# The prologue of a fused attention and MLP kernel: loads in order of use, a plain fp32 low-rank path, and another order of the first products

## The chip, the cores and the metric

The kernel runs on one core of one Trainium2 chip. The metric is device time in microseconds (us) of one launch. A launch has five engines with queues of their own: TensorE (PE: matmuls and transposes through an identity matrix), VectorE (DVE), ScalarE (ACT), GpSimd (POOL) and SyncE (SP), which here issues DMAs only. ACT and POOL issue some DMAs too. Each engine works its queue strictly in order; waits on semaphores tie them together.

## The reference

```python
# attention without softmax, per batch b (8) and head h (8): seq 576, head_dim 64
kv  = einsum('bhsd,bhse->bhde', k, v)
out = einsum('bhsd,bhde->bhse', q, kv)
x   = out / sqrt(mean(out*out, -1) + 1e-6) * g_norm          # then laid out as (8, 576, 512)
# block 1: low rank over the sequence (U 576x32, V 32x576), then an MLP 512 -> 2048 -> 512
u = x + (x.transpose(0,2,1) @ U @ V).transpose(0,2,1)
x = u + maximum(u @ w_ch1, 0) @ w_ch2
# block 2: h = gelu(x @ w_in), 1024 wide, halves u and v; v layer-normed, mixed over the
# sequence by w_sg (576x576) + b_sg; result x + (u * v) @ w_out
```

All inputs and the output are fp32.

## The kernel before, in words

The work is staged. The attention is cut into 32 units; unit m is one pair of heads of one batch (four units to a batch). For each unit PE multiplies k by v (`k_v`, L1439), transposes q (`q_transposed`, L1423), multiplies q by kv (`attention`, L1450 and L1452). ACT copies the result out of PSUM, squares it (L736) and takes a root (L740); DVE sums (L1011) and scales (L1018) to the normalised tile y. Then comes the low-rank part: PE forms a = U^T y (`low_rank`, L1458), DVE splits a into a high and a low part (`a_split`), and PE transposes y and adds V^T a (`u_transposed`, L1423 and L1469); ACT moves that to SBUF with g_norm (`u_evacuated`, L756), and SP stores it to DRAM (`store_u`, L388).

The MLP matmuls are run as three products of high and low parts in the type fp32r (L1418, L1419, L1420: hi by hi, hi by lo, lo by hi), and blocked in seven combined products in place of eight. So activations and weights need sums and differences first (`x_sum`, `w1_sums`), a rounded high part from ACT (`x_high` L771, `w1_high` L761) and a low part from DVE (`x_low` L1073, `w1_low` L1046). The up projection of batch t is a tile of 56 steps; a step is six matmuls; 14 steps are a group of the weight w_ch1 (four groups, 0 to 3). Between the steps of tile t the units of batch t+1 are worked at fixed places: after step 0 of the first tile the attention of unit 4 and k by v of unit 5; in every group low rank after step 7, `u_transposed` after step 10, the next unit's attention and k by v after step 13.

Before the first tile lies the prologue: units 0 to 3, the preparation of weight group 0, and k by v of unit 4. Its order is written out by hand in one loop `for m in range(HP)` on each engine. The raw k, v and q of units 0 to 4 come over SP's queue (q of unit 0 over ACT's), U, V and w_ch1 over POOL's. POOL issues w_ch1 in three parts: part 0 is group 0, part 1 is group 1, part 2 is groups 2 and 3; each part is eight DMAs, released by a count of finished k by v products. The sums of weight groups 0 and 1 are made by DVE, those of groups 2 and 3 by POOL. In SP's queue the loads of unit 5 (k and v, then q in 32-column blocks, L376) stand between the store of unit 0 and the stores of units 1 to 3. The first low part of an activation (`x_low(0, 0, 0)`) waits for the stores of units 0 and 1, because it overwrites what they read.

After the up projection come the down projection and block 2; they are not touched.

## Time and profile before

| what | value |
|---|---|
| median of three timed runs | 1295.93 us (1294.95 to 1296.66) |
| the profiled execution: its own time, and its span | 1293.79 us, 1292.0 us |
| PE busy | 1261.8 us, 98% of the span |
| DVE, ACT, POOL busy | 824.7 us, 543.8 us, 101.3 us |
| first matmul of the kernel, first up-projection product | 7.34 us, 45.93 us |
| attention of unit 5 (after step 13 of the first tile) | 67.14 us |
| read from and written to device memory | 109.47 MB, 66.06 MB |

The span is the time between the first and the last instruction in the trace; the execution's own time is what the timer gives around it. A share of busy time is a mean over all stages. The stage at issue here is the first 5% of the span.

### The profile page before, as it was taken

What the parts mean: (1) busy time and instruction counts of PE and PEld (TensorE: products, weight loads), DVE (VectorE), ACT (ScalarE), POOL (GpSimd) and SP (SyncE); (2) the same over time, 40 slices, a digit from 0 to 9 for tenths busy, and PEclk for the clock granted to TensorE, in tenths of its full rate; (3) what the DMA queues carried; (4) which work ended last, traced back from release to release, by engine and by line L of the source; (5) the groups of instructions that cost most, each with busy time, mean ns of one, the idle gap of its engine ahead of it and who ended that gap; (6) DMA issues with size and microseconds to landing.
All of it is one profiled execution on the core that took longest, in us unless ns stands there. A gap on an engine that the chain in (4) does not pass through costs nothing.

```text
span 1292.0 us, 21466 instructions
## 1 busy us (share of the span) xinstructions
PE 1261.8 (98%) x8311; PEld 1221.4 (95%) x8311; DVE 824.7 (64%) x1196; ACT 543.8 (42%) x867; POOL 101.3 (8%) x107
## 2 busy tenths in 40 slices
PE   5799999999999999999999999999999999999998
PEld 5699999999999999999999999998898998998987
DVE  4886465645555558998888889976634535336343
ACT  4565454445455445654535444534322212223121
POOL 7210000000000000000000000002302012022000
PEclk9899999999999999999999999999999999999999
DMA  9555665655565456671735446362342241340321
GB/s 236 131 154 154 176 164 157 156 147 156 173 166 157 129 189 242 215 260 62 265 101 191 170 154 225 100 196 57 96 85 66 62 113 50 72 111 31 57 58 41
DMA packets 285365, 178.61 MB, mean 138 GB/s; under 512 B 197456, under 2 KB 255840, under 8 KB 285296
## 3 DMA queue, kind: packets, MB, share of 16 engines
q1 hardware_dynamic: 282336, 172.82, 46.3%
q0 software_dynamic: 1600, 4.56, 1.3%
q8 instruction: 45, 0.74, 0.2%
q10 hardware_dynamic: 1360, 0.30, 0.1%
q14 instruction: 24, 0.20, 0.0%
HBM read 109.47 MB, written 66.06 MB: 136 GB/s over the span
## 4 chain that ended last, share of the span: by engine, by line
PE 93%; DVE 3%; issue 1%; ACT 1%; SPq 1%; DMA 0%; POOL 0%; DVEq 0%; ACTq 0%; POOLq 0%
PE ps L1418 28%; PE ps L1420 28%; PE ps L1419 27%; PE ps L1439 3%; PE ps L1450 2%; PE ps L1423 2%; PE ps L1458 1%; PE ps L1681 1%; PE ps L1684 1%; PE ps L1469 1%; PE ps L1452 1%; DVE w_lo L1180 0%; SPq L376 0%; DVE y L1018 0%; DVE x_lo L1073 0%
## 5 line engine op out<-in xcount | busy, mean ns | idle before, releaser
L1418 PE MATMUL ps<-x_hi,w 128*128 128x288 f32 x896 | 268.0, 299 | 3.5 <-DVE x_lo L1073 2.7
L1419 PE MATMUL ps<-x_lo,w 128*128 128x288 f32 x896 | 264.6, 295 | 0.0
L1420 PE MATMUL ps<-x_hi,w 128*128 128x288 f32 x896 | 264.3, 295 | 0.0
L1418 PE MATMUL ps<-r_hi,w_hi 128*128 128x384 f32 x672 | 224.6, 334 | 0.1
L1420 PE MATMUL ps<-r_hi,w_lo 128*128 128x384 f32 x672 | 224.5, 334 | 0.0
L1419 PE MATMUL ps<-r_lo,w_hi 128*128 128x384 f32 x672 | 224.5, 334 | 0.0
L880 ACT ACTIVATE r_hi<-hb 128x768 fp32r<-128x768 f32 x168 | 142.4, 848 | 168.5 <-PE ps L1420 164.7
L1418 PEld LDWEIGHTS ps<-x_hi,w 128*128 128x128 f32 x896 | 168.5, 188 | 5.6 <-issue 4.3
L1420 PEld LDWEIGHTS ps<-x_hi,w 128*128 128x128 f32 x896 | 168.8, 188 | 0.0
L1419 PEld LDWEIGHTS ps<-x_lo,w 128*128 128x128 f32 x896 | 168.7, 188 | 0.0
L1208 DVE TENSOR_TENSOR r_lo<-hb,r_hi 128x768 fp32r<-128x768 f32 x120 | 114.5, 955 | 30.0 <-ACT r_hi L880 30.0
L1418 PEld LDWEIGHTS ps<-r_hi,w_hi 128*128 128x128 f32 x672 | 126.2, 188 | 0.4 <-DVE r_lo L1206 0.4
L1420 PEld LDWEIGHTS ps<-r_hi,w_lo 128*128 128x128 f32 x672 | 126.2, 188 | 0.0
L1419 PEld LDWEIGHTS ps<-r_lo,w_hi 128*128 128x128 f32 x672 | 126.2, 188 | 0.0
L780 ACT ACTIVATE h_st<-ps 128x576 f32<-128x576 f32 x128 | 81.4, 647 | 55.7 <-PE ps L1420 51.2
L1084 DVE TENSOR_TENSOR h_st<-ps,h_st 128x576 f32<-128x576 f32 x96 | 71.9, 750 | 46.9 <-PE ps L1420 46.6
L1355 DVE SCALAR_TENSOR_TENSOR vs<-ps,glcol,bias_bc 128x576 f32<-128x576 f32 x32 | 26.1, 816 | 86.3 <-PE ps L1684 86.3
L1418 PE MATMUL ps<-ws_hi,vn_hi 128*128 128x288 f32 x256 | 75.6, 295 | 0.0
L1418 PE MATMUL ps<-x_hi,wu_hi 128*128 128x288 f32 x256 | 75.6, 295 | 0.0
L1420 PE MATMUL ps<-x_hi,wu_lo 128*128 128x288 f32 x256 | 75.5, 295 | 0.0
L1420 PE MATMUL ps<-ws_hi,vn_lo 128*128 128x288 f32 x256 | 75.4, 295 | 0.0
L1419 PE MATMUL ps<-ws_lo,vn_hi 128*128 128x288 f32 x256 | 75.4, 294 | 0.0
(156 smaller groups left out, 2347.1 us busy)
## 6 DMA issues: line engine op xcount, KB each, us to landing
hT_scratch<-h_st SPq DMA_DIRECT2D x64, 576.0 KB, 4.6
hb<-hT_scratch SPq DMA_DIRECT2D x24, 1536.0 KB, 7.5
uT_scratch<-x_raw SPq DMA_DIRECT2D x32, 288.0 KB, 2.3
x_st<-uT_scratch SPq DMA_DIRECT2D x24, 384.0 KB, 3.5
x2T_scratch<-x_st SPq DMA_DIRECT2D x24, 384.0 KB, 7.0
x_raw<-x2T_scratch SPq DMA_DIRECT2D x8, 1152.0 KB, 5.6
xt_in<-x2T_scratch SPq DMA_DIRECT2D x144, 64.0 KB, 2.5
k_raw<-in_k SPq DMA_DIRECT2D x64, 128.0 KB, 4.0
```

Of the source, the lines that this page charges most:

```text
L780: nc.scalar.activation(h_st[:, g % 2, :, {0: 0, 1: 3, 2: 1, 6: 2}[idx], :], ps[:, o:o + 2, 0:SH], ACT.Copy).then_inc(s_cp, 1)
L880: nc.scalar.activation(r_hi[:, n % RING], piece(h_source(i), q_), ACT.Relu if i in (3, 6) else ACT.Copy).then_inc(s_hhi, 1)
L1084: nc.vector.tensor_tensor(c, ps[:, o:o + 2, 0:SH], c, ALU.add).then_inc(s_ad, 1)
L1208: ins = nc.vector.tensor_tensor(lo, x, hi, ALU.subtract)
L1355: nc.vector.scalar_tensor_tensor(vs[:, c % 2, :].rearrange("p (a m) -> p a m", a=2), us_tile(c), glcol[:, c:c + 1], bias_bc[:].rearrange(" ...
L1418: mm(dst, ws[0], xs[0], start=first, stop=False, skip_group_check=chained)
L1419: mm(dst, ws[0], xs[1], start=False, stop=False, skip_group_check=chained)
L1420: return mm(dst, ws[1], xs[0], start=False, stop=last, skip_group_check=chained)
L1423: return mm(dst, src, identF[:], is_transpose=True, start=start, stop=stop)
L1439: ins = mm(ps[:, bx, at_:at_ + P], k_raw[n][:, j], v_raw[n][:, :, j, :], start=(j == 0), stop=(j == NJ - 1))
L1450: ins = mm(ps[:, bx, j * P:(j + 1) * P], qT[:, j], kv[:], start=True, stop=True)
L1452: mm(ps[:, by, 0:P], qT[:, JM], kv[:], start=True, stop=True).then_inc(s_out, 1)
```

## The change

Only the prologue and the first tile change. Seven things:

1. PE runs 12 transposes of the identity before it has data (`WARM`), and in each unit the transpose of q now comes before k by v. ACT takes a root of a constant right after its first two DMA issues, and q of units 0 and 1 are issued by ACT, q of unit 2 by POOL.
2. SP loads k and v of units 0, 1 and 2 first; unit 3 waits for the k by v of unit 1 (two finished).
3. POOL issues, after the first k by v: q of unit 2, V, then part 0 of w_ch1. Part 1 waits for four finished k by v as against three, part 2 for six as against four.
4. The low rank of units 0 to 3 runs in plain fp32 (`low_rank_first`, `a_split_first`): five matmuls of 128x128 on y itself by U repeated three times (`U_rep`). The high and low parts of y, the copy of a's second half and its addition are gone for these four units.
5. Attention of unit 4 comes before the first product, k by v of unit 5 behind step 5, and its evacuation is spread over the first steps (`first_steps`).
6. On DVE the first activation sums are interleaved with the normalisation of unit 4; `w1_low` of group 0 comes in the same loop.
7. SP stores units 0 and 1 before it loads k and v of unit 5, then units 2 and 3, then q of unit 5. POOL's sums of group 2 also wait for DVE's sums of group 1.

```diff
-            load_next(HP + 1)
-            for r in range(1, HP):
-                store_u(0, r)
+            store_u(0, 1)
+            load_kv((HP + 1) // HP, (HP + 1) % HP, HP + 1, 0)
+            store_u(0, 2)
+            store_u(0, 3)
+            load_q_blocks(HP + 1)
...
+            pool.wait_ge(s_kv, 1)
+            for h in range(2):
+                pool.dma_start(q_raw[2][:, 0:JM, h, :], ...).then_inc(s_q[2], 16)
...
             pool.wait_ge(s_kv, 1)
             load_w1(0, slice(0, 2))
-            pool.wait_ge(s_kv, 3)
+            pool.wait_ge(s_kv, HP)
             load_w1(1, slice(2, 4))
-            pool.wait_ge(s_kv, HP)
+            pool.wait_ge(s_kv, HP + 2)
             load_w1(2, slice(4, NPAIR))
+            pool.wait_ge(s_wsum[1], 4)
...
+            def a_split_first(m):
+                a = ps[:, 3, 0:P]
+                dve.wait_ge(s_a, m + 1)
+                nc.vector.tensor_copy(a_aug[:], a).then_inc(s_ahi, 1)
+                dve.wait_ge(s_ahi, m + 1)
+                o = slice(R, 2 * R)
+                nc.vector.tensor_tensor(a_aug[o, :], a[o, :], a_aug[o, :].bitcast(F32), ALU.subtract).then_inc(s_alo, 1)
...
+            def low_rank_first(m):
+                pe.wait_ge(s_y, m + 1)
+                for j in range(NJ):
+                    ins = mm(ps[:, 3, 0:P], U_rep[:, j], y_first[m % 3][:, j], start=(j == 0), stop=(j == NJ - 1))
+                ins.then_inc(s_a, 1)
...
+            for n in range(WARM):
+                ins = transpose(ps[:, 4, 0:P], identF[:], True, True)
             q_k_v_first(0)
...
-                if first and k == 0:
-                    attention_and_next(m)
+                if first and k == 5:
+                    pe.wait_ge(s_o, 2 * (HP + 1))
+                    k_v(HP + 1, BY, 1, 2, P)
```

On SP the place is the end of the prologue's queue, from q of unit 4 on. `uT_scratch` rows are the stores of units, `k_raw` and `v_raw` the loads of unit 5, `q_blk` its q. Before:

```order
L366 DMA q_raw<-in_q 64x2x64
L388 DMA uT_scratch<-x_raw_79 128x2x288 [waits uT_evacuated]
L351 DMA k_raw<-in_k 128x4x64 [waits kv_done]
L351 DMA k_raw<-in_k 128x4x64
L354 DMA k_raw<-in_k 64x2x64
L356 DMA v_raw<-in_v 128x2x256
L358 DMA v_raw<-in_v 64x2x64
L376 DMA q_blk<-in_q 32x18x32 [waits qT_done]
L376 DMA q_blk<-in_q 32x18x32 x3
L388 DMA uT_scratch<-x_raw_79 128x2x288 [waits uT_evacuated] x3
```

And after:

```order
L369 DMA q_raw<-in_q 64x2x64
L391 DMA uT_scratch<-x_raw_79 128x2x288 [waits uT_evacuated] x2
L354 DMA k_raw<-in_k 128x4x64 [waits kv_done]
L354 DMA k_raw<-in_k 128x4x64
L357 DMA k_raw<-in_k 64x2x64
L359 DMA v_raw<-in_v 128x2x256
L361 DMA v_raw<-in_v 64x2x64
L391 DMA uT_scratch<-x_raw_79 128x2x288 [waits uT_evacuated] x2
L379 DMA q_blk<-in_q 32x18x32 [waits qT_done]
L379 DMA q_blk<-in_q 32x18x32 x3
```

The second store now stands ahead of nine loads, and q of unit 5 behind all four stores.

On POOL the place is from the identity matrix on; `w_raw_59` is the raw weight of group 0, `w_raw_60` that of groups 1 to 3. Before:

```order
L646 DMA U_raw<-in_moe_U 128x4x32
L647 DMA U_raw<-in_moe_U 64x32
L649 DMA V_raw<-in_moe_V 32x576 x4
L656 DMA w_raw_59<-in_moe_w_ch 128x2x128 [waits kv_done]
L656 DMA w_raw_59<-in_moe_w_ch 128x2x128 x7
L656 DMA w_raw_60<-in_moe_w_ch 128x2x128 [waits kv_done]
```

And after:

```order
L651 DMA U_raw<-in_moe_U 128x4x32
L652 DMA U_raw<-in_moe_U 64x32
L659 DMA q_raw_90<-in_q 128x4x64 [waits kv_done]
L659 DMA q_raw_90<-in_q 128x4x64
L660 DMA q_raw_90<-in_q 64x2x64
L662 DMA V_raw<-in_moe_V 32x576 x4
L669 DMA w_raw_59<-in_moe_w_ch 128x2x128 [waits kv_done]
L669 DMA w_raw_59<-in_moe_w_ch 128x2x128 x7
```

Seven issues (three of q, four of V) now stand between the first k by v and the first weight DMA, where there was none.

On DVE the place is the end of the prologue, from the sum over the squares of unit 3 on. Before:

```order
L1022 TENSOR_TENSOR y_hl<-y,y_hl 128x5x128 [waits y_hi_ready]
L1053 TENSOR_TENSOR x_raw_79<-x_raw_79 128x576 [waits uT_evacuated]
L1026 TENSOR_TENSOR part<-ps,part 128x128 [waits a_part]
L1028 CAST a_aug<-part 128x128 [waits a_sum]
L1031 TENSOR_TENSOR a_aug<-part,a_aug 32x128 [waits a_hi_ready]
L1046 TENSOR_TENSOR w_0_55<-w_raw_59,w_0_55 128x1792 [waits w1_hi_ready]
L1073 TENSOR_TENSOR x_lo_77<-x_raw_79,x_hi 128x576 [waits uT_stored1,uT_stored0,x_hi_ready]
L1057 TENSOR_TENSOR x_raw_79<-x_raw_79 128x576 [waits u_sums_ready,uT_evacuated]
```

And after:

```order
L1048 TENSOR_TENSOR y_92<-y_92,rstd 128x640 [waits rstd_ready]
L1089 TENSOR_TENSOR w_0_55<-w_raw_59,w_0_55 128x1792 [waits w1_hi_ready]
L1096 TENSOR_TENSOR x_raw_79<-x_raw_79 128x576 [waits uT_evacuated]
L1066 CAST a_aug<-ps 128x128 [waits a_done]
L1069 TENSOR_TENSOR a_aug<-ps,a_aug 32x128 [waits a_hi_ready]
L1116 TENSOR_TENSOR x_lo_77<-x_raw_79,x_hi 128x576 [waits uT_stored1,uT_stored0,x_hi_ready]
L1100 TENSOR_TENSOR x_raw_79<-x_raw_79 128x576 [waits u_sums_ready,uT_evacuated]
L1116 TENSOR_TENSOR x_lo_77<-x_raw_79,x_hi 128x576 [waits x_hi_ready]
L1041 TENSOR_REDUCE ssum<-sq 128x10 [waits squares_ready]
```

The low part of y (L1022) is gone, the split of a has two instructions in place of three, the second weight low part has moved ahead of the last split, and the sum for unit 4 has moved in among the activation sums.

## Rows read from the trace of the kernel before

**Rows 1.** Waits of PE, whole span: what it waited for, us, times, longest.

```profile
PE ps L1439 <- DMA v_raw<-in_v: 7.3, 1, 7.3
PE ps L1450 <- ACT qT L710: 5.8, 4, 2.1
...
PE ps L1418 <- DVE x_lo L1073: 2.7, 1, 2.7
PE ps L1458 <- DVE y_hl L1022: 2.3, 1, 2.3
```

**Rows 2.** Windows: length, busy PE, PEld, DVE, ACT, POOL, PEclk, DMA share, GB/s.

```profile
14.00:15.00 1.00, 1.00 (x7) 1.00 (x7) 0.00 (x0) 0.85 (x3) 1.00 (x2) 0.54 0.97 266
...
67.00:100.00 33.00, 32.88 (x260) 32.67 (x259) 25.76 (x31) 21.76 (x36) 5.86 (x4) 1.00 0.56 158
```

**Rows 3.** Timeline of PE: start, us, engine, line, operation, tiles, [idle before].

```profile
7.34 2.47 PE L1439 MATMUL ps<-v_raw,k_raw 128*128 128x128 f32 x10 [7.34 <-DMA v_raw<-in_v]
...
45.93 0.58 PE L1418 MATMUL ps<-x_hi,w 128*128 128x288 f32 x1 [2.73 <-DVE x_lo L1073]
...
67.14 1.05 PE L1450 MATMUL ps<-kv,qT 128*128 128x128 f32 x8
...
69.77 0.29 PE L1418 MATMUL ps<-x_hi,w 128*128 128x288 f32 x1
...
75.37 0.29 PE L1418 MATMUL ps<-x_hi,w 128*128 128x288 f32 x1
```

**Rows 4.** Timeline of POOL: its DMA issues, and its first weight sum.

```profile
3.64 0.92 POOL L646 DMA_DIRECT2D U_raw<-in_moe_U  x1
4.55 0.55 POOL L647 DMA_DIRECT2D U_raw<-in_moe_U  x1
5.10 1.98 POOL L649 DMA_DIRECT2D V_raw<-in_moe_V  x4
10.11 5.67 POOL L656 DMA_DIRECT2D w_raw<-in_moe_w_ch  x8 [3.03 <-PE ps L1439]
...
26.90 5.95 POOL L656 DMA_DIRECT2D w_raw<-in_moe_w_ch  x8 [0.16 <-issue]
54.34 1.29 POOL L286 TENSOR_TENSOR w_raw<-w_raw 128x512 f32<-128x512 f32 x1 [21.50 <-PE ps L1420]
```

**Rows 5.** Tile w_raw, 0 to 60 us: time from issue to landing.

```profile
DMA to landing us min/median/max: 3.7/5.3/8.1
```

**Rows 6.** Groups of DVE, 0 to 46 us: busy us, mean ns, idle before.

```profile
L1046 DVE TENSOR_TENSOR w<-w_raw,w 128x1792 fp32r<-128x1792 f32 x2 | 4.1, 2026 | 0.6 <-ACT w L761 0.5
L1018 DVE TENSOR_TENSOR y<-y,rstd 128x640 f32<-128x640 f32 x4 | 3.3, 825 | 0.1
L1011 DVE TENSOR_REDUCE ssum<-sq_first 128x10 f32<-128x640 f32 x4 | 3.3, 815 | 3.8 <-ACT sq_first L736 3.8
L1031 DVE TENSOR_TENSOR a_aug<-part,a_aug 32x128 fp32r<-32x128 f32 x4 | 1.1, 281 | 0.1
L1073 DVE TENSOR_TENSOR x_lo<-x_raw,x_hi 128x576 fp32r<-128x576 f32 x1 | 0.8, 757 | 1.7 <-DMA uT_scratch<-x_raw 1.7
L286 DVE TENSOR_TENSOR w_raw<-w_raw 128x512 f32<-128x512 f32 x1 | 0.7, 686 | 0.0
```

**Rows 7.** Groups of ACT, 0 to 46 us.

```profile
L761 ACT ACTIVATE w<-w_raw 128x1792 fp32r<-128x1792 f32 x2 | 3.4, 1684 | 0.0
L756 ACT ACTIVATE x_raw<-ps,gcol 128x576 f32<-128x576 f32 x4 | 2.9, 727 | 2.3 <-PE ps L1469 2.3
L706 ACT ACT_TABLE_LOAD x1 | 1.3, 1283 | 10.8 <-PE ps L1423 10.8
L740 ACT ACTIVATE stdv<-ssum,eps_col 128x10 f32<-128x10 f32 x4 | 1.2, 303 | 3.9 <-DVE ssum L1011 3.9
```

**Rows 8.** Timeline of SP's queue: the issue of unit 5's q.

```profile
38.12 4.12 SPq L376 DMA_DIRECT2D q_blk<-in_q  x4
```

**Rows 9.** Timeline of DVE: the scaling of unit 4, with POOL at work.

```profile
54.52 1.79 DVE L1018 TENSOR_TENSOR y<-y,rstd 128x640 f32<-128x640 f32 x1
```

More of the change, by code:

```diff
@@ L54 @@
 NO = NJ
+WARM = 12
 NXT = 3
@@ L152, in build @@
     q_raw = [q_raw] + [at(f"q_raw{i}", [P, NJ, 2, HD], F32) for i in range(1, HP)]
[L153 removed]
+    y_first = [at(f"y{i}", [P, NJ, P], F32) for i in range(1, 3)] + [y]
     sq_first = at("sq_first", [P, NJ, P], F32)
[L155 to L156 removed]
+    U_rep = at("U_rep", [P, NJ, 4 * R], F32)
     assert cursor[0] <= phase_end
+    V_raw = at("V_raw", [P, S], F32, offset=x_hi_off + 2 * SH * 4)
+    U_raw = at("U_raw", [P, NJ, R], F32, offset=x_hi_off + 3 * 2 * SH * 4)
     wsize = FH * DH * 4
@@ L787, in x2_high, with load_q @@
                 nc.scalar.activation(x2_hi[par][:, :, 0:n], x2_raw[:, :, 0:n], ACT.Copy).then_inc(s_x2hi, 1)
-            for h in range(2):
-                act.dma_start(q_raw[0][:, 0:JM, h, :], q[0, h, 0:SM, :].rearrange("(j p) d -> p j d", p=P)).then_inc(s_q[0], 16)
-            act.wait_ge(s_zero, 1 + 3 * HP)
-            act.dma_start(q_raw[0][0:ST, JM, :, :], q[0, 0:2, SM:S, :].rearrange("h p d -> p h d")).then_inc(s_q[0], 16)
+            def load_q(m):
+                for h in range(2):
+                    act.dma_start(q_raw[m][:, 0:JM, h, :], q[0, 2 * m + h, 0:SM, :].rearrange("(j p) d -> p j d", p=P)).then_inc(s_q[m], 16)
+                if m == 0:
+                    act.wait_ge(s_zero, 1)
+                    nc.scalar.activation(stdv[:, 0:1], eps_col[:], ACT.Sqrt).then_inc(s_pass, 1)
+                    act.wait_ge(s_zero, 2 + 3 * HP)
+                act.dma_start(q_raw[m][0:ST, JM, :, :], q[0, 2 * m:2 * m + 2, SM:S, :].rearrange("h p d -> p h d")).then_inc(s_q[m], 16)
+            for m in range(2):
+                load_q(m)
             for n in range(2):
                 act.dma_start(gcol[HD * n:HD * (n + 1), :], g_norm.rearrange("(p o) -> p o", o=1)).then_inc(s_g, 16)
-            act.wait_ge(s_zero, 3 * HP + 6)
             q_copy(0, 0, first=True)
@@ L817, in _, with first_steps @@
             u_evacuated(2, 2, 4, 0, -1)
-            a_part(3, 3)
             x_high(0, 0, 1)
+            attn_copy(HP, BX, BY)
             u_evacuated(3, 3, 4, 0, -1)
-            for idx in range(2, NI):
-                x_high(0, 0, idx)
+            squares(HP, sq)
             X_HIGH_AT = (26, 34, 53)
             X_HIGH_THEN = (1, 2, 3, 6)
+            def first_steps():
+                x_high(0, 0, 2)
+                copied(0, 1)
+                std(HP)
+                x_high(0, 0, 3)
+                copied(0, 3)
+                x_high(0, 0, 4)
+                y_high(HP)
+                x_high(0, 0, 5)
+                copied(0, 5)
+                kv_copy(HP + 1, BY, P)
+                x_high(0, 0, 6)
             def up_tile(t, par, first=False, end=False):
-                for k in range(STEPS):
+                if first:
+                    first_steps()
+                for k in range(6 if first else 0, STEPS):
                     g, idx, s_ = step(k)
@@ L1103, in _ @@
                 kv_copy(m + 1, 2)
+                if m == HP - 1:
+                    a_split_first(m - 1)
                 normalise(m, ym)
-                if m:
-                    a_split(m - 1, 3)
-                y_low(m, ym)
+                if m == 0:
+                    low_rank_factors()
+                elif m < HP - 1:
+                    a_split_first(m - 1)
                 if m == 1:
                     w1_sums(dve, nc.vector, 0)
-                if m == 2:
-                    w1_low(0)
+                elif m > 1:
+                    w1_low(m - 2)
             x_sum(0, 0, 1)
-            a_split(3, 3)
-            w1_low(1)
+            a_split_first(3)
             x_low(0, 0, 0)
-            for idx, low_ in ((2, 1), (6, 2), (4, 3)):
-                x_sum(0, 0, idx)
-                x_low(0, 0, low_)
+            x_sum(0, 0, 2)
+            x_low(0, 0, 1)
+            sums(HP, sq)
+            x_sum(0, 0, 6)
+            x_low(0, 0, 2)
+            normalise(HP)
+            x_sum(0, 0, 4)
+            y_low(HP)
+            x_low(0, 0, 3)
+            x_low(0, 0, 4)
             w1_sums(dve, nc.vector, 1)
@@ L1123, in up_tile @@
             def up_tile(t, par, first=False, end=False):
-                for k in range(STEPS):
+                for k in range(5 if first else 0, STEPS):
                     g, idx, s_ = step(k)
@@ L1139, in up_tile @@
                         a_split(m, BX)
-                    if k in X_LOW_THEN[2 if first else 0:]:
+                    if k in X_LOW_THEN[3 if first else 0:]:
                         x_low(t, par, 2 + X_LOW_THEN.index(k))
@@ L1485, in _ @@
                 if m > 1:
+                    if m == 2:
+                        pe.wait_ge(s_low, 2)
+                    else:
+                        pe.wait_ge(s_uev, m - 2)
                     u_transposed(m - 2, 4, y_first[m - 2])
@@ L1509, in attention_step @@
                 m = HP * (t + 1) + r
-                if first and k == 0:
-                    attention_and_next(m)
+                if first and k == 5:
+                    pe.wait_ge(s_o, 2 * (HP + 1))
+                    k_v(HP + 1, BY, 1, 2, P)
                 if at_ == LOW:
```

75 lines of the change are left out of this document (40 added, 35 removed).

## The prediction, made before the changed kernel had run

> **What bounds the kernel now.** I read the waits of PE first, then the windows, then the timelines and groups of each engine over the first 70 us. The waits of PE [rows 1] show the only sizeable idle time of the launch: 7.3 us until the first k and v have landed, 5.8 us for the copy of transposed q, 2.7 us in one piece ahead of the first up-projection product, 2.3 us for the low rank of unit 4. From 67 us on PE is full: 32.88 of 33.00 us, at granted clock 1.00 [rows 2]. So what is saved before the attention of unit 5, at 67.14 us [rows 3], goes through to the end of the launch one for one, and nothing else can be saved. I therefore forecast one moment, the start of that attention, and carry its shift to the end.
>
> **How the early part hangs together.** The first product starts at 45.93 us [rows 3]. The reader is to see in its row that PE came free 2.73 us earlier and was released by a low part x_lo on DVE, and in DVE's group of that operation that DVE itself had waited 1.7 us for the store of the activation [rows 6]. That store was late because in SP's queue it stood behind the nine loads of unit 5, the four of q alone taking 4.12 us to issue from 38.12 us on [rows 8]. Further back it is a chain over DVE and ACT: the sums of weight group 0, then by turns the reduction of a unit's squares, its root, its evacuation and a weight high part on ACT, and a weight low part on DVE. PE mostly waits for that.
>
> **The change, part 1: when weight group 0 lands.** Before, POOL was released by the first k by v at 10.11 us and issued the eight DMAs in 5.67 us [rows 4], 0.71 us each, so the last began at 15.1; with the median of 5.3 us to landing [rows 5] it had landed at 20.4. DVE waited for nothing before its first sum [rows 6].
>
> After, the first k by v ends a little earlier. It took 2.47 us at the low clock level from 7.34 us on [rows 3]. Now the transpose of q and at best a PE at the high level come first; k's tail no longer waits for all 13 fills. I bound the release by 9.1 us (matmuls at the high level, half of 2.47) and 10.9 us (low level, transposes 0.8 us before them) and take 9.8. Then POOL issues q of unit 2, whose three DMAs I price like those of U, 0.92 + 0.92 + 0.55, and V, 1.98 [rows 4]: 4.4 us together, to 14.2 us. The last of the eight weight DMAs begins 4.96 us later, at 19.2, and lands 3.7 to 8.1, median 5.3 us after that [rows 5]: 22.9 to 27.3, taken as **24.5 us**. DVE will have finished the split of unit 0's a by about 21.5 us and will then stand at this wait, with every later DVE instruction queued behind it: the reduction, copy of kv and scaling of unit 2, and through them PE's attention of unit 3. This is the new wait that the change adds, and the first place where I expect its gain to be given back in part.
>
> At this place a rule of the Trainium skill speaks against the change. The row first: eight POOL issues took 5.67 us and another eight 5.95 us with DVE busy nearly throughout [rows 4]. "SBUF — State Buffer", section "SBUF: two separate sides", says that a DMA from GpSimd's queue has its descriptors written by the GpSimd cores, and that a DVE copy from SBUF to SBUF can lock them out for as long as it runs. By that rule the moved q and V could be held by each of the three new copies of U; by the rows one issue is lengthened by 5% at most.
>
> **Part 2: from the weight to the first product.** On the path from 24.5 us stand, with durations from [rows 6, 7]: the four sums of group 0, 4 x 0.686 less their overlap, 2.5; the reduction of unit 2, 0.8; ACT's root, evacuation of unit 0 and weight high part, 0.30 + 0.73 + 1.68 = 2.7; DVE's weight low part, 2.0; reduction of unit 3, 0.8; again root, evacuation, high part, 2.7; low part, 2.0; the sum for activation 1, 0.75; the split of unit 3's a, two instructions at 0.28, 0.55; PE's five transposes and two matmuls for unit 3, 1.0. Together 15.9 us, so the first product at **40.4 us**, 5.5 us earlier. What went out beside that path: per unit a high part and a copy on ACT, a low part (128x640, as the 0.825 of L1018) and an addition on DVE, four units, 3.3 + 1.2 us of DVE time of which some 4 us lay on the old path. The stores of units 0 and 1 are issued by about 34.5 us, so the 1.7 us wait goes; next late is the split of unit 3's a, by which DVE stands before its first x_lo. The fp32 low rank costs PE about what k by v costs, which is beside the DVE path and priced at nothing; if that cover went, four times 0.3 us. The attention of unit 4 runs in PE's wait, at nothing too.
>
> **Part 3: from the first product to the attention of unit 5.** Before: 67.14 - 45.93 = 21.2 us. PE's own work there is 14 steps, and a step takes (75.37 - 69.77) / 7 = 0.80 us at full clock [rows 3], 11.2 us; with k by v, low rank and the transposes of unit 4 about 14.1 after the change. DVE needs more: evacuation of unit 3 on ACT, 0.7; eight activation sums and low parts at 0.7 to 0.757, 5.8; reduction, reciprocal and scaling of unit 4, 1.9; ACT's two high parts that stand between, 1.3; y's low part 0.8; the sums of group 1, 2.6; the transpose of q, one h addition, 1.4; split of a, 0.8; then on PE the transposes of unit 4 and three steps, 3.4. That is 18.7 by the row durations; I take 18.5, since neighbours overlap by some 0.07 us each. So **58.9 us**, 8.2 us earlier than 67.14. PE idles about 4 us in this stretch, in pieces of one to two us.
>
> The clock: in the window 14 to 15 us the granted clock is 0.54 of 2.4 GHz [rows 2], that is mostly the 1.2 GHz level, after PE had stood idle about 2 us before its first attention; the first product after 2.73 us of idle took 0.58 in place of 0.29 us [rows 3]. The new gaps are shorter, so a fall costs at most one or two of them, and most of it lies under DVE's path: between 0 and 1.7 us, taken as nothing beyond the rounding above.
>
> **Part 4: what comes back.** POOL's sums of group 2 began at 54.34 us [rows 4], and DVE's scaling of unit 4 at 54.52 took 1.79 us [rows 9] in place of 0.825 [rows 6]. They went on together, and PE's 2.3 us wait for unit 4's low part [rows 1] came of it. After the change part 2 is issued only from the k by v of unit 5 on, about 47 us, in 5.95 us, and lands near 58. The sums then run beside DVE's last weight low part of group 1 and the scaling of unit 5, which PE needs at steps 15 and 21. Each DVE instruction with two SBUF inputs may lose up to 1 us there, from two to four of them; PE's slack is about 1 us. Between 0 and 4 us, taken as **1.0**.
>
> **Sum.** 8.2 - 1.0 = 7.2 us. The profiled execution took 1293.79 us around a span of 1292.0; it would take 1286.6. The median of the timed runs is 2.1 us above the profiled one, so on that scale 1295.93 - 7.2 = **1288.7 us**.
>
> **Rivals.** (A) POOL's queue is later than I take it: release at 10.9, landing after 8.1 us, some issues held up. Weight group 0 is then there at 29 us and the gain shrinks by 4.5 to 2.7 us, 1293.2 us. For it: landings of up to 8.1 us, with the DMA engines at a share of 0.97 in the window 14 to 15 us [rows 2]. Against it: the same queue now carries fewer bytes in the same time. (B) It lands before DVE comes for it at 21.5 us, and no sum on POOL costs PE anything: 3.0 + 1.0 more, a gain of 11.2, 1284.7 us. For it: POOL's DMAs compete with less, since unit 3 and half of w_ch1 wait. Against it: it needs a landing faster than the quickest seen, or a q of unit 2 that issues faster than U. (C) Slower than before: weight groups 2 and 3, now released by the sixth k by v in place of the fourth, come too late for step 28. Part 2's last DMA begins near 52.5 us; at worst it lands at 60.7; four sums on POOL take 5.2 us alone [rows 4] and about twice that in collision with DVE, so they end between 63 and 71. Then 1.68 and 2.03 us [rows 6, 7] must fit in before step 28 at about 74 us. The point from which it decides is sums ending after 70; to turn the result over, at 1298.6 us (2.7 above), they would have to end at 80. Against it: nothing in the rows reaches that far. (D) The 12 transposes do not do what their name says. No stretch of this trace has transposes alone. PE would then stay at 1.2 GHz through the first k by v, the release is 10.4 to 10.9 us, and the gain is 6.4 us, 1289.5 us: inside my case. The Trainium skill, "TensorE: Matmul & The Clock Gate", "Part 4: PE-mode transpose", says that such transposes do not count as a busy PE; by that rule the granted clock stays low until after the first matmuls on real data.
>
> **Numbers.** My case, with D in it: 68%, 1286.4 to 1290.9 us. A: 16%. B: 10%. C or another late piece: 6%. A measurement here can tell 0.2%, 2.6 us, from no change. Faster: 68 + 12 of A + 10 = 90%; within 0.2%: 4 of A + 1 of C = 5%; slower: 5%. The range leaves out the far end of B and C: 1284.8 to 1292.8 us.
>
> **What would show it.** In the profile after: POOL's first w_raw issue at about 14 us; DVE idle before its first w_raw sum, ended by the DMA, for up to 3 us; the first product near 40.4 us, released by PE's own queue or by the split of a; no wait of x_lo for uT_scratch; the attention that follows step 13 near 59 us; PE full from there except near steps 15 and 21. It is wrong if PE waits for w1's low part at step 28, if the first product comes after 44 us, or if the shift at 67 us is not the shift at the end.

## The result, and the profile after

The changed kernel ran in 1287.68 us (median of 4 runs, 1286.45 to 1289.27) against 1295.44 us (4 runs, 1294.64 to 1296.66) for the kernel before on the same chip: a ratio of 0.994, interval 0.9923 to 0.9957, or 7.8 us less. The forecast was 1288.7 us, the range 1284.8 to 1292.8.

Waits of PE after, whole span (what it waited for, us, times, longest), against [rows 1]:

```profile
PE ps L1502 <- issue: 4.3, 2, 2.4
PE ps L1475 <- POOL identF L649: 3.4, 1, 3.4
PE ps L1470 <- DVE x_lo L1116: 2.4, 3, 1.6
```

The waits for the copy of transposed q and for the high and low parts of y have left the top of the list. Apart from the 3.4 us until POOL has made the identity matrix, the largest single one is now 2.4 us, before an attention. Timeline of PE after, the lines that answer to [rows 3]:

```profile
7.66 2.12 PE L1491 MATMUL ps<-v_raw,k_raw 128*128 128x128 f32 x10
...
28.80 1.13 PE L1502 MATMUL ps<-kv,qT 128*128 128x128 f32 x8 [2.42 <-issue]
...
33.23 1.32 PE L1491 MATMUL ps<-v_raw,k_raw 128*128 128x128 f32 x10
...
41.66 0.32 PE L1470 MATMUL ps<-x_hi,w 128*128 128x288 f32 x1
...
60.15 1.05 PE L1502 MATMUL ps<-kv,qT 128*128 128x128 f32 x8
```

The first product is at 41.66 us, 4.27 earlier than before, the attention of unit 5 at 60.15, 6.99 earlier. POOL after, answering to [rows 4]:

```profile
10.07 1.53 POOL L659 DMA_DIRECT2D q_raw<-in_q  x2 [4.54 <-PE ps L1491]
11.60 0.61 POOL L660 DMA_DIRECT2D q_raw<-in_q  x1
12.20 2.01 POOL L662 DMA_DIRECT2D V_raw<-in_moe_V  x4
14.20 5.68 POOL L669 DMA_DIRECT2D w_raw<-in_moe_w_ch  x8
...
49.44 5.96 POOL L669 DMA_DIRECT2D w_raw<-in_moe_w_ch  x8 [18.23 <-PE ps L1491]
...
63.00 1.30 POOL L289 TENSOR_TENSOR w_raw<-w_raw 128x512 f32<-128x512 f32 x1 [7.60 <-DMA w_raw<-in_moe_w_ch]
```

Weight group 0 is issued from 14.20 us on, and POOL's sums of group 2 begin at 63.00 in place of 54.34. On DVE [rows 6, 9] one sees the new wait, and that the work on unit 4 is stretched no more:

```profile
24.84 0.69 DVE L289 TENSOR_TENSOR w_raw<-w_raw 128x512 f32<-128x512 f32 x1 [2.52 <-DMA w_raw<-in_moe_w_ch]
...
34.59 0.47 DVE L1138 COPY kv<-ps 64x64 f32<-64x64 f32 x2 [1.06 <-PE ps L1491]
...
35.70 0.29 DVE L1066 CAST a_aug<-ps 128x128 fp32r<-128x128 f32 x1 [0.64 <-PE ps L1527]
...
40.70 0.76 DVE L1116 TENSOR_TENSOR x_lo<-x_raw,x_hi 128x576 fp32r<-128x576 f32 x1
...
46.28 0.82 DVE L1048 TENSOR_TENSOR y<-y,rstd 128x640 f32<-128x640 f32 x1
```

The scaling of unit 4 takes 0.82 us (before 1.79), and x_lo waits for no store. The split of unit 5's a, at 70.59 us, is still stretched (1.28 us in place of 0.28), with POOL's sums beside it. Windows after (length, busy PE, PEld, DVE, ACT, POOL, PEclk, DMA share, GB/s), against [rows 2]:

```profile
30.00:31.00 1.00, 0.69 (x5) 0.44 (x3) 0.63 (x3) 1.00 (x2) 1.00 (x2) 0.50 0.84 269
60.00:93.00 33.00, 32.90 (x261) 32.70 (x260) 26.60 (x31) 21.73 (x36) 12.90 (x8) 1.00 0.66 173
```

From 60 us on PE is full again, with POOL at work for 12.90 of 33 us. At 30 us its granted clock is 0.50, the 1.2 GHz level, right after the wait of 2.42 us.

**From 60 us to the end.** The profiled execution of after took 1288.74 us around a span of 1286.9. That is 5.1 less span than before's 1292.0, though the attention of unit 5 had moved by 7.0. The shift was still 6.7 us at a wait of PE in block 2 for the low part ws_lo, of the same length in both (2.14 and 2.15 us): it ends at 888.73 us before and at 882.00 after. One window behind it, in before and then in after:

```profile
890.00:892.00 2.00, 2.00 (x18) 2.00 (x17) 1.42 (x2) 0.83 (x2) 0.00 (x0) 1.00 0.01 2
```

```profile
884.00:886.00 2.00, 2.00 (x10) 2.00 (x10) 0.97 (x2) 0.18 (x1) 0.00 (x0) 0.50 0.03 8
```

The code there is the same. In this execution of after the clock was at its lower level and 10 matmuls passed in 2 us in place of 18; the shift fell to 5.2 us. Of the fourteen traces of this study eight show the fall at that place and six do not. Kernels built on the changed one and kernels built on the one before are among both, so I take it to belong to an execution and not to the change; no kernel was traced both with the fall and without it. From the end of that wait to the end of the span take 404.8 to 404.9 us with the fall and 403.3 to 403.4 without, so by itself it makes single executions differ by some 1.5 us. So below, early moments are read in the traces and totals only in medians.

### The profile page after: what moved, and what is told of

It reads as the page before. It is cut to its first block, busy times and chain, and to the rows that moved or that the text cites. A ratio compares the mean times of both kernels' runs of the same rounds, so it can differ in the third digit from the quotient of the medians.

```text
span 1286.9 us, 21517 instructions
## 1 busy us (share of the span) xinstructions
PE 1263.7 (98%) x8343; PEld 1222.5 (95%) x8343; DVE 817.9 (64%) x1189; ACT 539.3 (42%) x859; POOL 104.2 (8%) x111
## 4 chain that ended last, share of the span: by engine, by line
PE 94%; DVE 3%; DMA 1%; issue 1%; POOL 1%; ACT 1%; ACTq 0%; DVEq 0%
PE ps L1470 28%; PE ps L1472 28%; PE ps L1471 28%; PE ps L1491 2%; PE ps L1502 2%; PE ps L1475 2%; PE ps L1510 1%; PE ps L1747 1%; PE ps L1750 1%; PE ps L1521 1%; PE ps L1504 0%; DMA w_raw<-in_moe_w_ch 0%; POOL w_raw L669 0%; DMA q_raw<-in_q 0%; DVE x_lo L1116 0%
## 5 line engine op out<-in xcount | busy, mean ns | idle before, releaser
L1471 PE MATMUL ps<-x_lo,wu_hi 128*128 128x288 f32 x256 | 76.1, 297 | 0.0
```

What stands on the lines that cost most here:

```text
L1471: mm(dst, ws[0], xs[1], start=False, stop=False, skip_group_check=chained)
```

## The experiments

FP is the first product, A5 the attention of unit 5, each from the profiled execution. Kernels of one group below shared a chip; the kernel before took 1295.0, 1295.0, 1295.4 and 1295.1 us there.

**1. SP's order undone.** The changed kernel with part 7's queue of SP as before.

```diff
             store_u(0, 0)
-            store_u(0, 1)
-            load_kv((HP + 1) // HP, (HP + 1) % HP, HP + 1, 0)
-            store_u(0, 2)
-            store_u(0, 3)
-            load_q_blocks(HP + 1)
+            load_next(HP + 1)
+            for r in range(1, HP):
+                store_u(0, r)
```

> The changed kernel with only SP's queue as before: the loads of unit 5's k, v and q stand again between the store of unit 0 and the stores of units 1 to 3. My account (DVE's path sets the first product, and the wait for the store had been taken off it): k and v of unit 5 are issued from 35.3 us (released by the k by v of unit 4), q until about 42.5, the store of unit 1 lands near 45.5, so the first x_lo comes at 45.5 in place of 40.7 and the first product at 46.3 to 46.8 in place of 41.66; the attention of unit 5 at 64.0 to 65.0 in place of 60.15, the launch 4 to 5 us longer. Rival (the new order on SP is worth little, because DVE is late anyway): under 1.5 us.

1288.91 us (8 runs, 1287.6 to 1291.69), ratio 0.9958 (0.9947 to 0.9968). FP 42.06, A5 59.92. DVE:

```profile
41.16 0.76 DVE L1114 TENSOR_TENSOR x_lo<-x_raw,x_hi 128x576 fp32r<-128x576 f32 x1 [2.29 <-DMA uT_scratch<-x_raw]
```

The wait for the store is back, 2.29 us long, at the place I said. Yet the time rises by only 1.2 us (1288.91 - 1287.68, intervals overlapping), not by the 4 to 5 expected. I had moved the 4.12 us of q's issue [rows 8] over unchanged and it took 2.21, and k and v of unit 5 were issued from 32.71 us, not 35.3. This trace has no clock fall between 28 and 41 us; against the one trace of the changed kernel without a fall (experiment 9: 39.71, 58.20) the first product is 2.35 us later and A5 1.7.

**2. No transposes.** `WARM = 12` becomes `WARM = 0`.

> The changed kernel without the 12 identity transposes at the start. My account: they do not raise the granted clock, since the first k by v after them still took 2.12 us; so POOL's first issue stays at 10.1 us, DVE's first weight sum at 24.8, the attention of unit 5 at 60.15, all within 0.3 us, launch within 0.5 us. Rival (they bring PE to 2.4 GHz earlier than real matmuls alone would): the attention of unit 0 and k by v of unit 1 run at the 1.2 GHz level, 1.7 and 2.1 us in place of 1.1 and 1.2, and the launch is 1 to 2 us longer.

1286.93 us (4 runs, 1286.38 to 1289.29), 0.9937 (0.9922 to 0.9952): no slower. PE:

```profile
6.77 1.30 PE L1475 MATMUL ps<-identF,q_raw 128*128 128x128 f32 x5 [6.77 <-DMA q_raw<-in_q]
7.86 2.34 PE L1491 MATMUL ps<-v_raw,k_raw 128*128 128x128 f32 x10
10.77 2.07 PE L1502 MATMUL ps<-kv,qT 128*128 128x128 f32 x8 [0.57 <-DVE kv L1138]
```

PE stays at the lower level through the attention of unit 0 and most of the k by v of unit 1 (2.02 us), and the attention of unit 1, at the high level again with 1.13 us, comes at 16.77 in place of 14.53 us. But DVE's first weight sum is at 25.18 (24.84), behind a wait of 2.36 us for the DMA, FP at 41.70, A5 at 60.19. Most of what PE loses ends in front of weight group 0.

**3. Fp32 products in place of the transposes.**

```diff
-WARM = 12
+WARM = 6
-                ins = transpose(ps[:, 4, 0:P], identF[:], True, True)
+                ins = mm(ps[:, 4, 0:P], identF[:], identF[:], start=True, stop=True)
```

> The changed kernel with six plain fp32 matmuls of the identity by itself in place of the 12 transposes at the start; they should fill PE for about the same 2.8 us. If transposes do not count for the clock and products do: the first k by v runs at least partly at 2.4 GHz, 1.1 to 1.7 us in place of 2.12, POOL's first issue comes 0.4 to 1.0 us earlier than 10.07 and with it the landing of weight group 0, DVE's first weight sum (24.84) and the attention of unit 5 (60.15). Rival (the clock answers to time, not to the kind of work): nothing moves by more than 0.3 us.

1287.81 us (4 runs, 1286.56 to 1289.28), 0.9945 (0.993 to 0.996). PE:

```profile
6.52 1.33 PE L1475 MATMUL ps<-identF,q_raw 128*128 128x128 f32 x5 [0.20 <-DMA q_raw<-in_q]
7.64 1.32 PE L1491 MATMUL ps<-v_raw,k_raw 128*128 128x128 f32 x10
```

The first k by v ran at the high level (1.32 us against 2.12), POOL's first issue behind it was at 9.26 us (10.07), DVE's first sum came at 24.12, FP at 39.72, A5 at 58.23, with no clock fall on the way. I would have put those two us down to the kind of matmul, but the next kernels say otherwise (experiment 4, and the changed kernel run again).

**4. Weight group 0 issued early.** q of unit 2 goes to ACT's queue, V to SP's, and ACT loads g_norm after its first copies, so POOL has nothing ahead of the weight.

```diff
-            for h in range(2):
-                pool.dma_start(q_raw[2][:, 0:JM, h, :], ...)        # and its tail
-            for n in range(4):
-                pool.dma_start(V_raw[R * n:R * (n + 1), :], V[:, :])
...
                 if m == HP - 1:
+                    for n in range(4):
+                        sp.dma_start(V_raw[R * n:R * (n + 1), :], V[:, :])
...
-            for m in range(2):
+            for m in range(3):
                 load_q(m)
```

> The changed kernel with V issued by SP in its idle time after unit 2's k and v, and q of unit 2 issued by ACT behind q of unit 1 (g_norm after the first copies), so that POOL issues weight group 0 at once after the first k by v. My account (the landing of weight group 0 is what holds DVE from 22.3 to 24.84 us): POOL's first w_raw issue at 10.1 in place of 14.20, landing near 20.5, DVE's wait of 2.52 us gone, and also PE's 2.4 us gap before the attention of unit 3 with the fall of its clock after it, 1 us more: attention of unit 5 at 56.6 to 57.7 in place of 60.15, launch 2.5 to 3.5 us shorter than the changed kernel. Rival (bytes, not issues, are the limit: the DMA engines have a share above 1 up to 26 us): weight group 0 then lands later than 22.3 or pushes k and v of units 1 and 2 late, and under 1 us is gained.

1286.66 us (5 runs, 1285.55 to 1287.73), 0.9935 (0.9922 to 0.9949). FP 40.01, A5 58.50. PE, then DVE:

```profile
3.39 2.82 PE L1470 MATMUL ps<-identF 128*128 128x128 f32 x12 [3.39 <-POOL identF L651]
6.71 0.77 PE L1470 MATMUL ps<-identF,q_raw 128*128 128x128 f32 x5 [0.50 <-DMA q_raw<-in_q]
7.31 1.28 PE L1486 MATMUL ps<-v_raw,k_raw 128*128 128x128 f32 x10
```

```profile
18.86 0.46 DVE L1076 CAST V_aug<-V_raw 128x576 fp32r<-128x576 f32 x1 [2.86 <-DMA V_raw<-in_moe_V]
...
23.59 0.69 DVE L289 TENSOR_TENSOR w_raw<-w_raw 128x512 f32<-128x512 f32 x1
```

The weight was issued at 8.89 us and DVE no longer waits for it. It waits 2.86 us for V instead, which stands earlier in its queue, and its first weight sum is only 1.25 us earlier, or 0.51 against the 24.10 of experiment 9. The launch is 1.0 us shorter than the changed kernel's 1287.68, so my expectation of 2.5 to 3.5 us less fell. The PE rows answer experiment 3 too: after transposes alone the five of q ran in 0.77 us, the high level.

**5. SP's order alone, in the kernel before.** The edit of experiment 1 the other way round.

```diff
-            load_next(HP + 1)
-            for r in range(1, HP):
-                store_u(0, r)
+            store_u(0, 1)
+            load_kv((HP + 1) // HP, (HP + 1) % HP, HP + 1, 0)
+            store_u(0, 2)
+            store_u(0, 3)
+            load_q_blocks(HP + 1)
```

> The kernel before with one part of the change: SP stores units 0 and 1 ahead of the loads of unit 5, and issues q of unit 5 last. If this part takes away the 1.69 us for which DVE waited for the store and nothing else, the first x_lo comes at 43.2 to 43.4 in place of 45.02, the first product at 44.1 to 44.4 in place of 45.93, and the launch is 1.5 to 2 us shorter. Rival (the stall only moves to unit 4's chain behind the first product): the attention of unit 5 stays at 67.1, launch within 0.5 us.

1293.75 us (10 runs, 1292.57 to 1295.21), 0.9992 (0.9982 to 1.0001). FP 44.87 (45.93 before), A5 65.90 (67.14). PE:

```profile
44.87 0.58 PE L1420 MATMUL ps<-x_hi,w 128*128 128x288 f32 x1 [1.72 <-DVE x_lo L1075]
```

PE waits 1.72 us for x_lo where it waited 2.73: the store's wait is gone, 1.1 us. The expected 1.5 to 1.8 us at the first product came out as 1.06. The medians differ by 1.3 us, but the interval of the ratio reaches 1.0001, so the total alone does not tell this from nothing. With experiment 1 from the other side, part 7 is worth 1.2 to 1.7 us at A5.

**6. The fp32 low rank alone, in the kernel before.** Part 4 of the change and nothing else.

```diff
-                    low_rank(m - 1, 3)
+                    low_rank_first(m - 1)
...
-                    a_split(m - 1, 3)
-                y_low(m, ym)
+                    a_split_first(m - 1)
```

> The kernel before with another part alone: the low rank of units 0 to 3 in plain fp32, with no high and low parts of y and no copy and addition of a for them. My account (about 4 us of DVE's path went with them): the k by v of unit 4 at 29.5 to 30.5 in place of 32.60, the first product 2.5 to 4 us earlier than 45.93 with the old order on SP, the launch 2.5 to 4 us shorter. Rival (PE's fp32 matmuls or the old order on SP take it back): under 1.5 us.

1295.11 us (10 runs, 1293.84 to 1296.18), 0.9997 (0.9987 to 1.0006), FP 45.82: nothing in the median and at FP, where I expected 2.5 to 4. A5 is at 65.86, 1.3 us before the 67.14 of the kernel before, which the interval does not exclude. PE, then DVE:

```profile
34.35 0.77 PE L1432 MATMUL ps<-identF,q_raw 128*128 128x128 f32 x5 [2.46 <-DMA q_raw<-in_q]
...
45.82 0.58 PE L1427 MATMUL ps<-x_hi,w 128*128 128x288 f32 x1 [2.15 <-DVE x_lo L1083]
```

```profile
37.21 0.29 DVE L1036 CAST a_aug<-ps 128x128 fp32r<-128x128 f32 x1 [2.80 <-PE ps L1483]
...
41.91 0.29 DVE L1036 CAST a_aug<-ps 128x128 fp32r<-128x128 f32 x1 [3.31 <-PE ps L1483]
```

The work taken off DVE did bring the attention of unit 3 forward by 1.1 us. Then PE stood 2.46 us at q of unit 4, which SP had finished issuing at 28.28 us (25.79 before), its clock went down to 0.50, and DVE waited 2.80 and 3.31 us for PE. The saved DVE time turned into waiting, first for data and then for PE at the lower clock.

**7. The bytes as before.** The changed kernel with parts 1 and 2 of w_ch1 released by the old counts.

```diff
-            pool.wait_ge(s_kv, HP)
+            pool.wait_ge(s_kv, 3)
             load_w1(1, slice(2, 4))
-            pool.wait_ge(s_kv, HP + 2)
+            pool.wait_ge(s_kv, HP)
```

> The changed kernel with parts 1 and 2 of w_ch1 released by three and four finished k by v products, as before, in place of four and six. If the order of bytes matters (the DMA engines are full until 26 us): part 1 is issued right behind part 0 from about 20 us, q and k of unit 3 and all of unit 4 land 2 to 4 us later, PE waits for them, and the attention of unit 5 comes 1.5 to 4 us after 60.15. If DVE's path hides it (my account: data were there when PE asked in the changed kernel): within 0.7 us. The sums of group 2 on POOL stay behind DVE's sums of group 1 in both.

1290.32 us (10 runs, 1288.67 to 1298.46), 0.9968 (0.9953 to 0.9984). FP 41.32, no later than with the new counts; PE's waits for q were 0.25 to 0.86 us. The loss comes behind it: A5 at 62.82, 21.5 us after FP. That is 2.7 us after 60.15, inside the range that I had given to the bytes, but for another cause. POOL, DVE and PE:

```profile
53.59 1.74 POOL L289 TENSOR_TENSOR w_raw<-w_raw 128x512 f32<-128x512 f32 x1 [22.16 <-DVE w_raw L294]
```

```profile
55.88 0.76 DVE L1058 CAST a_aug<-part 128x128 fp32r<-128x128 f32 x1
56.68 1.24 DVE L1061 TENSOR_TENSOR a_aug<-part,a_aug 32x128 fp32r<-32x128 f32 x1
```

```profile
58.07 0.41 PE L1475 MATMUL ps<-identF,y 128*128 128x128 f32 x2 [2.79 <-DVE a_aug L1061]
```

POOL's sums of group 2, early again, lie beside DVE's split of unit 4's a: 0.76 and 1.24 us where after has 0.23 and 0.28, and PE stands 2.79 us behind them, 1.5 more than in after. The clock fell behind that gap (0.50 from 60 to 62 us), which is the rest of the 3.0 us by which the stretch is longer. I had said that POOL's sums would stay behind DVE's sums of group 1; they did, and met the split instead. The two later releases together are worth 2.6 us, and not for the bytes; that it is the one of part 2 is read from where the loss lies.

**8. K by v of unit 5 first.** `if first and k == 5:` becomes `if first and k == 0:`.

> The changed kernel with k by v of unit 5 behind the first product step in place of the sixth. Its v is issued until 38.5 us and lands near 43, so PE may wait 0.5 us at step 1; but DVE's low parts set the steps after it. My account: attention of unit 5 within 0.4 us of the 18.5 us after the first product, launch within 0.5 us. Rival (PE would stand at a late v with all products behind it): the first steps end 1 to 3 us later and so does the launch.

1288.23 us (4 runs, 1286.56 to 1290.91), 0.9947 (0.9928 to 0.9965). FP 40.91, A5 59.42, again 18.5 us apart. PE:

```profile
41.73 1.28 PE L1491 MATMUL ps<-v_raw,k_raw 128*128 128x128 f32 x10
...
59.42 1.05 PE L1502 MATMUL ps<-kv,qT 128*128 128x128 f32 x8
```

The product ran at once, with no wait for its data. Behind which step it stands makes no difference here, although part 2 of the weight, which this product releases, was issued at 43.30 us in place of 49.44: DVE sets the pace.

**9. The changed kernel again**, on the chip of experiments 10 and 11.

> The changed kernel once more, for its spread and a second trace. If the place where PE's granted clock falls is chance (in the first trace after the 2.4 us gap before the attention of unit 3, and again at 883 us): the attention of unit 5 between 58.2 and 60.3 us, and the transposes of w_sg near 882 with or without a fall of the clock, 1.6 us apart. If the fall after the gap belongs to the kernel: 60.1 again within 0.2 us.

1287.41 us (5 runs, 1286.9 to 1288.85), 0.9943 (0.9929 to 0.9956). PE:

```profile
28.06 1.13 PE L1502 MATMUL ps<-kv,qT 128*128 128x128 f32 x8 [1.21 <-issue]
...
39.71 0.31 PE L1470 MATMUL ps<-x_hi,w 128*128 128x288 f32 x1
...
58.20 1.05 PE L1502 MATMUL ps<-kv,qT 128*128 128x128 f32 x8
```

The same kernel, and the moments of experiment 3: its gap before the attention of unit 3 was 1.21 us in place of 2.42, the granted clock at 30 us was 1.00 in place of 0.50, and FP came 1.95 us earlier. Of these, 0.74 us were there at DVE's first weight sum (24.10), since the first k by v took 1.39 us in place of 2.12; the rest goes with the fall. That removes my reading of experiment 3.

**10. Low-rank factors late**, on top of experiment 4: DVE splits U and V at unit 1 in place of unit 0.

```diff
-                if m == 0:
-                    low_rank_factors()
-                elif m < HP - 1:
+                if 0 < m < HP - 1:
                     a_split_first(m - 1)
                 if m == 1:
+                    low_rank_factors()
                     w1_sums(dve, nc.vector, 0)
```

> As the kernel with the weights issued early (V on SP, q of unit 2 on ACT), and DVE prepares the low-rank factors from U and V in unit 1, between the split of unit 0's a and the sums of weight group 0, in place of unit 0, where it waited 2.86 us for V with the reduction of unit 1 behind it. My account (DVE's order, no longer POOL's issues, was the limit there): attention of unit 2 near 19 in place of 21.91, DVE's first weight sum at 21.8 to 22.8 in place of 23.59, first product 38.2 to 39.2, attention of unit 5 at 56.7 to 57.7 without a fall of the clock, launch 1 to 2 us shorter than the kernel with weights early and 2 to 3 below the changed one. Rival (q and v of units 1 to 3 arrive too late once DVE is faster, since the DMA engines are full): PE's waits on q_raw and v_raw grow by what DVE saves, launch within 0.5 us.

**1285.87 us** (5 runs, 1285.66 to 1287.14), 0.993 (0.9917 to 0.9944): the fastest median of the study, 1.5 us under the changed kernel on the same chip, with intervals that overlap, where I had expected 2 to 3. FP 39.19, A5 57.69. DVE, then PE:

```profile
22.43 0.69 DVE L289 TENSOR_TENSOR w_raw<-w_raw 128x512 f32<-128x512 f32 x1
```

```profile
22.46 0.45 PE L1469 MATMUL ps<-identF,y 128*128 128x128 f32 x2 [2.38 <-DVE V_aug L1080]
...
57.69 1.05 PE L1496 MATMUL ps<-kv,qT 128*128 128x128 f32 x8
...
70.43 0.41 PE L1469 MATMUL ps<-identF,y 128*128 128x128 f32 x2 [0.64 <-DVE a_aug L1056]
```

DVE waits for no weight and no V; now PE waits 2.38 us for the split of V, and its clock fell to 0.50 behind that gap. The last row is a wait that the changed kernel's own traces do not have: the split of unit 5's a took 0.91 and 1.27 us beside POOL's sums.

**11. POOL's sums late, in the kernel before.** One number.

```diff
-                pool.wait_ge(s_p, 2 * NI * (g - 2) + 4)
+                pool.wait_ge(s_p, 2 * NI * (g - 2) + 12)
```

> The kernel before with POOL's sums of weight groups 2 and 3 released eight steps later, nothing else. If their meeting with DVE's work on unit 4 cost what the changed kernel gained behind its first product: first product unchanged at 45.9, DVE's scaling of unit 4 back at 0.82 us, PE's waits of 2.32 and 0.71 us behind step 7 mostly gone, attention of unit 5 at 64.0 to 65.2 in place of 67.14, launch 2 to 3 us shorter. Rival (DVE is late there anyway): under 0.7 us. If the later sums are themselves missed, PE waits for a weight low part at step 28, near 79 us.

1290.63 us (8 runs, 1289.78 to 1292.06), 0.9968 (0.9957 to 0.9978): 4.7 us less in the medians from one number, where I had expected 2 to 3; the interval is 2.8 to 5.6, and the shift at A5 is 3.45 us. FP 46.26, A5 63.69, so 17.4 us apart where the kernel before has 21.2. DVE, then PE:

```profile
54.54 0.83 DVE L1018 TENSOR_TENSOR y<-y,rstd 128x640 f32<-128x640 f32 x1
55.28 0.75 DVE L1073 TENSOR_TENSOR x_lo<-x_raw,x_hi 128x576 fp32r<-128x576 f32 x1
56.17 0.82 DVE L1022 TENSOR_TENSOR y_hl<-y,y_hl 128x640 fp32r<-128x640 f32 x1
56.91 0.75 DVE L1073 TENSOR_TENSOR x_lo<-x_raw,x_hi 128x576 fp32r<-128x576 f32 x1
```

```profile
63.69 1.05 PE L1450 MATMUL ps<-kv,qT 128*128 128x128 f32 x8
```

Before, the same four DVE instructions took 1.79, 1.85, 1.88 and 1.84 us beside POOL's sums.

**12. Unit 3 first**, on top of experiment 10: PE takes q and k by v of unit 3 ahead of `u_transposed` of unit 0.

```diff
                     if m == 2:
+                        q_k_v_first(m + 1)
                         pe.wait_ge(s_low, 2)
...
-                q_k_v_first(m + 1)
+                if m != 2:
+                    q_k_v_first(m + 1)
```

> As the kernel with the factors late, and PE transposes q and multiplies k by v of unit 3 ahead of the transposes of unit 0, which waited 2.38 us for the low-rank factors with these behind them. My account (DVE then stood 1.26 us for kv of unit 3): that wait goes and PE has no gap over 1.5 us there, so the attention of unit 3 comes at 26.6 to 27.1 in place of 27.96, the first product at 37.8 to 38.3 in place of 39.19, the attention of unit 5 at 56.3 to 56.9 in place of 57.69, launch 0.8 to 1.5 us shorter. Rival (q of unit 3 lands at 24.2 us at the earliest, so bytes take over as the limit): under 0.4 us.

1287.91 us (5 runs, 1287.27 to 1289.19), 0.9945 (0.9931 to 0.9958). FP 40.75, A5 59.26. PE:

```profile
24.32 0.74 PE L1469 MATMUL ps<-identF,q_raw 128*128 128x128 f32 x5 [2.45 <-DMA q_raw<-in_q]
...
29.58 1.06 PE L1496 MATMUL ps<-kv,qT 128*128 128x128 f32 x8
```

PE does not wait for V's split any more, but 2.45 us for q of unit 3. The median is 2.0 us above that of experiment 10, on another chip and with overlapping intervals, where I had expected 0.8 to 1.5 less. A part of that may be this execution: its first k by v took 2.34 us and the attention of unit 0 2.08, both the low level, in spite of the transposes ahead of them. In this part of the launch each wait removed uncovers one of nearly the same length behind it, by turns for weight, V, its split and q.

## Why the forecast held, step by step

**What bounds the kernel: right.** PE is full from the attention of unit 5 on in both traces, and the shift of 7.0 us there was still 6.7 at 882 us. Of the rest of the difference between the two spans, 1.5 us is the clock fall behind it, which one execution had and the other had not.

**Part 1, the landing of weight group 0: right.** POOL's first weight issue was forecast at 14.2 and came at 14.20; DVE's first sum was forecast at 24.5 and came at 24.84, behind a wait of 2.52 us. That the 14.2 came out to the last digit is luck: POOL was released at 10.07, not 9.8, and q and V took 4.13 us, not 4.4. The rule of the Trainium skill that I weighed there, "SBUF — State Buffer", section "SBUF: two separate sides", by which DVE's copies hold up the descriptors of POOL's DMAs, did not show in these issues: q and V took 1.53 + 0.61 + 2.01 us, and the eight weight issues 5.68 us, before 5.67. The rule was hardly put to the test: the three copies of U ran at 8.37 us, ahead of POOL's release, and beside the issues DVE made two casts from SBUF to SBUF, 0.52 and 0.46 us long. What I did not see is how little lies behind this wait. Taking it away (experiment 4) gave 0.5 to 1.2 us at the first sum, and of rival B's 3.0 us nothing like that could be had, because V and DVE's own order come next.

**Part 2, the first product: late by 1.3 us (41.66 for 40.4).** The landing accounts for 0.3, the path for 0.9: 16.82 us in place of 15.9. The term that failed is the clock, which I took as nothing, with 1.7 as its upper end, because the new gaps were to be shorter. PE's clock fell after the gap of 2.42 us before the attention of unit 3; k by v of unit 4 was late, and DVE stood 1.06 and 0.64 us for PE. In the two traces without a fall on this path it took 15.61 us (experiment 9) and 15.60 (experiment 3). So the fall costs about 1.2 us when it comes, and the row durations of my sum were 0.3 too long. Another 0.7 us hangs on how early the clock rises at the start, through the landing. The two other credits of this part were measured apart. The store's wait (1.7 us) is worth 1.2 to 1.7 (experiments 1 and 5). The fp32 low rank, to which I gave "some 4 us" of DVE's path, is worth nothing at the first product of the kernel before and at most 1.3 us at A5 (experiment 6), since data and then PE set the time there. What it is worth in the changed kernel I did not measure; I take it from experiment 6 that it pays only together with the new order of the loads, which no run shows.

**Part 3, 18.5 us from the first product to the attention of unit 5: right in size, its cause not booked.** The stretch was 60.15 - 41.66 = 18.49 us, and 18.5 again in experiments 8 and 9. I had added up undisturbed row durations. That took the collision of POOL's sums with DVE out of the stretch, and I spoke of it only under what comes back. Experiment 11 shows that this is where that part of the gain is: with the sums of group 2 later and nothing else changed, the stretch in the kernel before falls from 21.2 to 17.4 us. Experiment 7 shows it from the other side: with the old releases put back, the changed kernel needs 21.5 us again, half of the 3.0 us more by the collision itself and the rest by the clock that falls behind it. The gain at the attention of unit 5 divides into 4.3 us up to the first product and 2.7 behind it (6.2 and 2.7 in the trace without a clock fall). Of the first of these, 1.2 to 1.7 us belong to part 7; how the rest divides among the order of the loads, the early transposes of q and the fp32 low rank is not shown.

**Part 4, what comes back: too high for this trace.** I took 1.0 us of 0 to 4. POOL did work for 12.90 us beside DVE between 60 and 93 us, with waits and stretched instructions there, but PE was busy for 32.90 of 33 us, and from A5 to the wait at 882 us only 0.3 was lost. That and the unbooked clock of part 2 nearly cancel, which is why the total is within 1.0 us (a gain of 7.2 forecast, 7.8 measured in the medians). This is luck: two of the terms were off by about 1 us each, and executions of one kernel differ by more than that. The collision itself is real, and costs more where A5 comes earlier. From A5 to the wait in block 2 passed 821.6 us before and 821.9 after, but 822.2 in experiment 9, 822.9 in experiment 10, 823.3 in experiment 3 and 823.4 in experiment 4; of the 1.3 us more in experiment 10, 0.64 is the last row shown there, behind the split that POOL's sums stretched. So below some 60 us the shift at A5 no longer goes through in full: of the 2.5 us that experiment 10 is ahead of the changed kernel there, 1.4 are left in block 2.

**The rivals.** A did not happen: the landing was within 0.4 us of the forecast. B did not happen; experiments 4 and 10 took its wait away and got at best 1.5 us under the changed kernel, with overlapping intervals. C did not happen: PE is full through step 28. D: transposes alone can raise the clock, as experiment 4 shows (the five of q in 0.77 us, k by v in 1.28), but not in every execution ahead of the first k by v: it took 1.39 us in experiment 9, 2.12 in after, and 2.34 in experiment 12, as without transposes. Without them the launch is no slower (experiment 2), and the wait for weight group 0 hides most of what PE loses. The Trainium skill, "TensorE: Matmul & The Clock Gate", "Part 4: PE-mode transpose", says that such transposes do not count as a busy PE; experiment 4's row speaks against it for the fp32 transposes here, and the measurement decides; the other traces alone would not settle it.

**Open.** What the fp32 low rank is worth inside the changed kernel, how the gain up to the first product divides among the parts other than 7, and what decides at which of two like gaps the clock falls. Not tried: the one-number edit of experiment 11 with the prologue of experiment 10.

## What to carry to other kernels

Before a start-up phase is rearranged, look behind it for instructions whose duration is twice that of their like elsewhere: here one number that moved POOL's work out of DVE's way gave about half of what the whole rearrangement gave (3.45 of 7.0 us at A5, 4.7 of 7.8 in the medians). A wait in a chain of loads is worth not its own length but its distance to the next wait behind it; price that one too. A shift goes through to the end only as far as no stretched instruction behind it becomes the late one. Where a forecast of a few us rests on one profiled execution, look for the places at which the clock may fall, and compare the moments ahead of them.

## What the runs showed of the hardware

- PE's granted clock fell to 0.50 (1.2 GHz) after gaps of 2.42 us (after), 3.20 us (experiment 4), 2.45 us (experiment 12) and 1.91 us (before, ahead of the attention at 29.65), and did not after 1.21 us (experiment 9), 1.91 us at the same attention in experiment 5, 2.32 us (before, ahead of the low rank at 59.94) and 3.35 us (experiment 5, ahead of 38.42). So in these traces the length of a gap alone does not tell whether the clock falls. In block 2 the same gap of 2.15 us was followed by a fall in eight traces and by none in six, at a cost of about 1.5 us.
- DVE instructions with two SBUF inputs beside POOL's sums took 1.79 to 1.88 us for what takes 0.75 to 0.83 alone; the small split of a took 0.76 and 1.24 us in place of 0.23 and 0.28. POOL's sum is stretched too, 2.03 and 3.07 us in experiment 11 against 1.29.
- The four DMA issues of unit 5's q took SP 4.12 us before, with the DMA engines at a share of 1.14 to 1.23, 2.21 us in experiment 1 at 0.68 to 0.81, and 2.99 us in after at 0.45 to 0.71: the same issues can cost twice as much, and the share alone does not order them.
